# A shorter lag between scores and transposes in an attention loop, with the P·V matmuls regrouped, on one Trainium2 core

## The chip, the cores and the metric

The kernel runs on one core of one Trainium2 chip. The time is the device time of one execution in microseconds (us). Engines are named as in the profile: PE is TensorE's matmul, PEld its weight load, DVE is VectorE, ACT is ScalarE, POOL is GpSimd, SP issues most of the DMAs.

## The reference, cut to what matters

```python
scores = scale * q @ k.T + bias[h]          # 4 batches x 8 heads, 576 x 576, head size 64
attn = exp(scores - max); attn /= attn.sum(-1) + 1e-9
x = attn @ v                                # rows of 8 heads x 64 = 512
logits = x @ w_gate                         # 8 experts
noisy = logits + log1p(exp(x @ w_noise)) * noise
# the two best experts of each of 2304 rows, weights by softmax over the two
out[row] += weight * (relu(x[row] @ w1[e]) @ w2[e])
```

`bias` comes from a small network over the relative position; it is the same for all batches.

## The kernel before, in words

The program has three stages: the bias table (to about 65 us of the span), attention (about 65 to 345 us), and the routing and the expert layers (the rest). The change touches only attention.

There are 32 heads (4 batches of 8). The 576 query rows of a head are cut into five tiles, four of 128 rows and one of 64, so there are TILES = 160 tiles. One loop over t = 0..159 stands in the program of each engine (PE L606, DVE L809, ACT L1108), and each engine works its own list in order; semaphores tie the lists together.

In iteration t PE issues, in this order:

- `qk(t)` (L542): six matmuls give the scores of tile t in `ps[t % 2]`. It waits until DVE is through with tile t-2.
- `pv`: the output of one head is the sum over five key tiles kt of V times the transposed probabilities. `PVAT` maps (t - VLAG) mod 5 to the key tiles done in that iteration. Before, each iteration does one key tile (4 records at L599). VLAG = NU + LT + 1 is 12.
- `logits`: once in 40 iterations the gate matmuls of a whole batch (L581).
- `flip(t - LT)`, with LT = 6 (L560): transposes of the probabilities of tile t-6 into the PSUM banks `pt[0]` (first half of the rows) and `pt[1]` (second half). The fifth tile of a head uses one bank, the head's number mod 2.
- `xtile`: after the fifth tile of some heads, four transposes of finished outputs (L548), into the bank that the fifth tile leaves free.

`flip` has these two waits; `pt` has one buffer for each bank, so the second is for the copies of the flip before:

```python
pe.wait_ge(norm_done, t + 1)
for bank in banks(t):
    if uses(bank, ("p", t)):
        pe.wait_ge(t_done[bank], uses(bank, ("p", t)))
```

DVE does in iteration t `evac0(t - LT - 1)` (L796, the copy of `pt[0]` to SBUF, which increments `t_done[0]`), then `ttr(t)` (L775, bias, scale and row maximum), then, where (t-2) mod 5 is 1, 3 or 4, `recip(t - 2)` (L786 and L788). ACT does `evac1(t - LT - 1)` (L1084, the copy of `pt[1]`), `expo(t - 1)` (L1069) and once a head `oevac` (L1097, the head's output, at OLAG). POOL normalises each tile (`norm`, L1228) once `recip` is through, and between the norms it splits the q and k of the head after the next (`high` L1207 and L1209, `qlow` L1214, `klow` L1220). The probabilities lie in ER = 7 buffers `E`.

After the loop each engine has a hand-written order for the last flips, the last three heads' P·V, the gate matmuls and the start of the routing (PE L626 to L647, DVE L860 to L875, ACT L1128 onward).

Of the kernel before, what the change touches and what calls it, by code (L numbers as in the profile page):

```python
# [22 lines left out]
B, H, S, D = 4, 8, 576, 64  # L23
# [3 lines left out]
NU = -(-S // P)  # L27
# [57 lines left out]


TILES = B * H * NU
LT, ER = 6, 7
VLAG = NU + LT + 1
PVAT = {kt: (kt,) for kt in range(NU)}  # L90
OLAG = VLAG + max(PVAT) + 1
GLAG = OLAG + 1
XT = 96
# [6 lines left out]
def banks(t):  # L100

    n, u = divmod(t, NU)
    return (0, 1) if u < NU - 1 else (n % 2,)


def xtile_with(t):

    n, u = divmod(t, NU)
    if u < NU - 1 or n % H in (0, 4) or n < 5:
        return None  # L110
    b, at = divmod(n - 5, H)
    return b, at - (at >= NX)
# [16 lines left out]
def uses(bank, e):  # L129

    return ORDER[bank].index(e)


def xbank(b, u):

    return [("x", b, u) in o for o in ORDER].index(True)


def build(nc, qT, kT, v, rtab, pcol, rcp8, w1c, b1c, w2b, wg, noise, mw1, mw2, consts, out, xs):
    ctx = ExitStack()  # L140
    with ctx:
# [361 lines left out]
        def _(pe):  # L503
# [26 lines left out]
            def part(half):  # L530
                return slice(half * D, (half + 1) * D)
# [18 lines left out]
            def flip(t):  # L550

                n, u = divmod(t, NU)
# [4 lines that stand above are left out]
                for kt in range(NU):  # L557
                    for half in range(2 if u < NU - 1 else 1):
                        bank = half if u < NU - 1 else n % 2
                        mm = nc.tensor.transpose(pt[bank][:, kt * D:(kt + 1) * D], E[t % ER][part(half), kt * P:(kt + 1) * P],  # L560
                                                 ident[part(half), part(half)])
                        if kt == NU - 1:
                            mm.then_inc(t_ready[bank], 1)

            def flip_x(u, bank):

                group, c = divmod(u, NX)
                for j in range(4):
                    mm = tr(bank[0:XT, j * P:(j + 1) * P], OT[:, group * 4 + j, c * XT:(c + 1) * XT], P)
                return mm  # L570

            def xtile(b, u):
                bank = xbank(b, u)
                pe.wait_ge(ot_done, b * H + (u // NX + 1) * 4)
                pe.wait_ge(t_done[bank], uses(bank, ("x", b, u)))
                flip_x(u, pt[bank]).then_inc(t_ready[bank], 1)
# [8 lines left out]
            def pv(n, kts):  # L585
                b, h = divmod(n, H)
                if kts[0] == 0:
                    for t in (n * NU + NU - 2, n * NU + NU - 1):
                        for bank in banks(t):
                            pe.wait_ge(t_done[bank], uses(bank, ("p", t)) + 1)  # L590
                    pe.wait_ge(v_loaded[n % 4], 16 * (n // 4 + 1))
                    if n >= 2:
                        pe.wait_ge(ot_done, n - 1)
                    if h == 1 and b:
                        pe.wait_ge(g_done, b)

                for kt in kts:
                    for half in range(2):
                        mm = nc.tensor.matmul(po[half * D:(half + 1) * D, n % 2, 0:HALF], vs[n % 4][:, kt, :],  # L599
                                              PT[n % 2][:, kt, half * HALF:(half + 1) * HALF],  # L600
                                              start=kt == 0, stop=kt == NU - 1)
                        if kt == NU - 1:
                            mm.then_inc(pv_half, 1) if half == 0 else mm.then_inc(pv_done, 1)

            pe.wait_ge(pt_zeroed, 1)
            for t in range(TILES):  # L606
                qk(t)
                if t >= VLAG and (t - VLAG) % NU in PVAT:
                    pv((t - VLAG) // NU, PVAT[(t - VLAG) % NU])
                b, at = divmod(t - GLAG - (H - 1) * NU, H * NU)  # L610
# [12 lines left out]
                                          start=True, stop=True)  # L623
                mm.then_inc(lt_ready, 1)

            flip(TILES - 6)  # L626
            xtile(*xtile_with(TILES - 6))
            pv(B * H - 3, (3, 4))
            flip(TILES - 5)
            pe.wait_ge(ttr_done, TILES - 1)  # L630
            pe.wait_ge(g_done, B - 1)
            pe.wait_ge(pid_done, 2)
            folded(range(CL), 0)
            pv(B * H - 2, (0, 1, 2))
            flip(TILES - 4)
            pv(B * H - 2, (3, 4))
            flip(TILES - 3)
            pe.wait_ge(ttr_done, TILES)
            pe.wait_ge(ot_done, B * H - 2)
            logits(range(H - 2), ps[1][:, 0, :])  # L640
            flip(TILES - 2)
            pe.wait_ge(ot_done, B * H - 1)
            logits([H - 2], ps[1][:, 0, :])
            flip(TILES - 1)
            xtile(*xtile_with(TILES - 1))
            pv(B * H - 1, range(NU))
            pe.wait_ge(ot_done, B * H)  # L647
            logits([H - 1], ps[1][:, 0, :]).then_inc(g_ready, 1)
# [92 lines left out]
        def _(dve):  # L741
# [48 lines left out]
            def evac0(t):  # L790
                n, u = divmod(t, NU)
                dve.wait_ge(t_ready[0], uses(0, ("p", t)) + 1)
                if n >= 2:
                    dve.wait_ge(pv_half, n - 1)
                    dve.wait_ge(pv_done, n - 1)
                nc.vector.tensor_copy(PT[n % 2][:, :, u * P:u * P + D], pt[0][:, 0:NU * D].rearrange("p (k s) -> p k s", k=NU))\  # L796
                    .then_inc(t_done[0], 1)
# [61 lines left out]

            dve.wait_ge(p_loaded, 32)  # L860
            dve.wait_ge(c2_loaded, CONSTS2)
            evac0(TILES - 7)
            recip(TILES - 2)
            evac0(TILES - 6)
            recip(TILES - 1)
            evac0(TILES - 5)
            copied(early, 0)
            evac0(TILES - 4)
            perturbed(early, 0)
            evac0(TILES - 3)  # L870
            evac0(TILES - 2)
            indexed(early)
            x_evac(*xtile_with(TILES - 1))
# [146 lines left out]
        def _(act):  # L1020
# [56 lines left out]
            def evac1(t):  # L1077
                n, u = divmod(t, NU)
                at = u * P + (D if u < NU - 1 else 0)
                act.wait_ge(t_ready[1], uses(1, ("p", t)) + 1)  # L1080
                if n >= 2:
                    act.wait_ge(pv_half, n - 1)
                    act.wait_ge(pv_done, n - 1)
                nc.scalar.activation(PT[n % 2][:, :, at:at + D], pt[1][:, 0:NU * D].rearrange("p (k s) -> p k s", k=NU),  # L1084
                                     ACT.Copy).then_inc(t_done[1], 1)

            def oevac(n):
                b, h = divmod(n, H)
                act.wait_ge(pv_half, n + 1)
                act.wait_ge(pv_done, n + 1)  # L1090
                if h == 0 and b:
                    act.wait_ge(g_ready, b)
                if h % 4 == 0 and b:
                    for u in range(h // 4 * NX, h // 4 * NX + NX):
                        bank = xbank(b - 1, u)
                        act.wait_ge(t_ready[bank], uses(bank, ("x", b - 1, u)) + 1)
                nc.scalar.activation(OT[:, h, :], po[:, n % 2, 0:HALF], ACT.Copy).then_inc(ot_done, 1)  # L1097

            def x_evac(b, u):
                act.wait_ge(t_ready[1], uses(1, ("x", b, u)) + 1)  # L1100
                act.wait_ge(x_stored, 32 * b)
                nc.scalar.activation(*x_rows(u, pt[1]), ACT.Copy).then_inc(t_done[1], 1)

            def last_x(i, bank):
                act.wait_ge(x_ready, i + 1)
                nc.scalar.activation(*x_rows(NX + i, bank), ACT.Copy).then_inc(x_done, 1)
# [13 lines left out]
            def softplus(cs, half):  # L1120
                act.wait_ge(lt_copied, half + 1)
                some = ez[:, :, :].rearrange("p (a c) e -> p a c e", a=2)[:, :, cs[0]:cs[-1] + 1, :]
                raw = logit[:, :, NE:16].rearrange("p (a c) e -> p a c e", a=2)[:, :, cs[0]:cs[-1] + 1, :]
                nc.scalar.activation(some, raw, ACT.Exp).then_inc(r_act, 1)
                act.wait_ge(r_act, 2 * half + 1)
                nc.scalar.activation(some, some, ACT.Ln, bias=1.0).then_inc(r_act, 1)

            evac1(TILES - 7)  # L1128
            expo(TILES - 1)
            x_evac(*xtile_with(TILES - 6))  # L1130
            oevac(B * H - 3)
            evac1(TILES - 5)
            evac1(TILES - 4)
            softplus(range(CL), 0)
            oevac(B * H - 2)
            evac1(TILES - 3)
            evac1(TILES - 2)
            evac1(TILES - 1)
            oevac(B * H - 1)
            last_x(0, po[:, 1, :])  # L1140
            softplus(range(CL, NT // 2), 1)
# [232 lines left out]
```

## Time and profile before

| what | us |
|---|---|
| median of 3 runs | 859.82 (858.33 to 860.89) |
| the profiled execution | 859.82 |
| its span, first to last instruction | 858.0 |
| PE busy | 794.0 (93%) |
| DVE, ACT, POOL busy | 502.0, 391.9, 384.0 |
| from 100 to 327 us: PE busy | 227.0 of 227.0, granted clock 1.00 |
| from 100 to 327 us: DVE, ACT, POOL busy | 192.4, 169.8, 184.4 |

The span is cut into 40 slices of 21.45 us in the page; slices 4 to 15 are attention. An engine's share over the whole span mixes the three stages, so the stage has to be read by itself. The profiled execution lies 1.8 us over its span; that part is outside the first and the last instruction.

### The profile page before, as it was taken

What the parts mean: (1) busy time and instruction counts of PE and PEld (TensorE: products, weight loads), DVE (VectorE), ACT (ScalarE), POOL (GpSimd) and SP (SyncE); (2) the same over time, 40 slices, a digit from 0 to 9 for tenths busy, and PEclk for the clock granted to TensorE, in tenths of its full rate; (3) what the DMA queues carried; (4) which work ended last, traced back from release to release, by engine and by line L of the source; (5) the groups of instructions that cost most, each with busy time, mean ns of one, the idle gap of its engine ahead of it and who ended that gap; (6) DMA issues with size and microseconds to landing.
All of it is one profiled execution on the core that took longest, in us unless ns stands there. A gap on an engine that the chain in (4) does not pass through costs nothing.

```text
span 858.0 us, 18369 instructions
## 1 busy us (share of the span) xinstructions
PE 794.0 (93%) x6558; PEld 614.7 (72%) x6558; DVE 502.0 (59%) x1201; ACT 391.9 (46%) x824; POOL 384.0 (45%) x439
## 2 busy tenths in 40 slices
PE   3986999999999999249999999999999999999994
PEld 1335665666666665249899899898898998988983
DVE  5987888888888885883533524435336235344310
ACT  3996777777777774413423323234224123232200
POOL 4006888788787872053232432342333324412212
PEclk9998999999999999669999999999999999999998
DMA  6786343353343235244262470461643714712122
GB/s 137 205 229 147 100 117 89 93 154 87 98 142 100 83 114 210 59 131 189 50 169 103 75 245 12 77 231 33 129 157 56 213 49 73 246 14 37 14 25 37
DMA packets 51174, 97.16 MB, mean 113 GB/s; under 512 B 12640, under 2 KB 21472, under 8 KB 51104
## 3 DMA queue, kind: packets, MB, share of 16 engines
q1 hardware_dynamic: 39920, 74.55, 28.5%
q0 software_dynamic: 10320, 21.41, 13.6%
q8 instruction: 42, 0.69, 0.3%
q10 hardware_dynamic: 864, 0.29, 0.2%
q14 instruction: 28, 0.23, 0.1%
HBM read 65.07 MB, written 20.53 MB: 100 GB/s over the span
## 4 chain that ended last, share of the span: by engine, by line
PE 85%; DVE 4%; DMA 4%; ACT 2%; issue 2%; POOL 1%; SPq 1%; POOLq 0%; DVEq 0%; ACTq 0%
PE ps L704 26%; PE po L719 24%; PE po L599 12%; PE ps L542 8%; PE pt L560 8%; PE pt L548 3%; DMA out_rows<-ys,iscat 2%; PE ps L522 1%; ACT work L1052 1%; ACT work L1045 1%; DVE work L760 1%; PE po L522 1%; DVE ohlo L940 1%; DMA w2blk<-in_w2b 1%; DMA qraw<-in_qT 1%
## 5 line engine op out<-in xcount | busy, mean ns | idle before, releaser
L704 PE MATMUL ps<-xT,whi 128*128 128x320 f32 x1024 | 176.1, 309 | 1.0 <-ACT xT L1152 1.0
L719 PE MATMUL po<-whi,hT 128*128 128x512 f32 x640 | 162.5, 398 | 0.0
L1163 ACT ACTIVATE hT<-ps 128x320 fp32r<-128x320 f32 x128 | 56.0, 437 | 231.8 <-PE ps L704 231.8
L704 PEld LDWEIGHTS ps<-xT,whi 128*128 128x128 f32 x1024 | 156.2, 187 | 1.8 <-issue 1.2
L987 DVE SCALAR_TENSOR_TENSOR hT<-ps,hT 128x320 fp32r<-128x320 f32 x128 | 62.9, 492 | 153.0 <-ACT hT L1163 153.0
L1228 POOL TENSOR_SCALAR work<-work,rcp 128x576 f32<-128x576 f32 (+1 forms) x160 | 118.2, 748 | 51.2 <-DVE rcp L788 51.2
L719 PEld LDWEIGHTS po<-whi,hT 128*128 128x128 f32 x640 | 118.1, 188 | 26.9
L1267 POOL DMA_INDIRECT out_rows<-ys,iscat x40 | 68.5, 1712 | 133.3 <-DMA out_rows<-ys,iscat 75.3
L775 DVE CUSTOM_DVE_ANT_0 ns<-ps,slab 128x576 f32<-128x576 f32 (+1 forms) x160 | 120.8, 756 | 11.3 <-PE ps L542 11.1
L1069 ACT ACTIVATE work<-ns,nmax 128x576 f32<-128x576 f32 (+1 forms) x160 | 122.6, 766 | 3.8 <-DVE nmax L775 3.3
L560 PEld LDWEIGHTS pt<-cst,work 64*128 64x128 f32 x1440 | 62.7, 139 | 73.9 <-issue 42.8
L599 PE MATMUL po<-work,vs 128*64 128x288 f32 x640 | 112.0, 433 | 0.1
L1254 POOL DMA_INDIRECT xg<-x_rows,igath x30 | 32.4, 1081 | 153.3 <-DVE ys L1002 80.1
L1002 DVE TENSOR_SCALAR ys<-po,wrow 128x512 f32<-128x512 f32 x40 | 30.0, 751 | 112.9 <-PE po L719 102.3
L704 PE MATMUL ps<-xT,wlo 128*128 128x320 f32 x512 | 95.7, 308 | 0.0
L1084 ACT ACTIVATE work<-pt 128x320 f32<-128x320 f32 x144 | 63.0, 437 | 65.5 <-PE pt L560 64.1
L560 PE MATMUL pt<-cst,work 64*128 64x64 f32 x1440 | 84.2, 233 | 5.0 <-DVE work L796 2.1
L796 DVE COPY work<-pt 128x320 f32<-128x320 f32 x144 | 70.7, 491 | 26.9 <-PE pt L560 24.9
L719 PE MATMUL po<-wlo,hT 128*128 128x512 f32 x320 | 81.1, 395 | 0.0
L806 DVE TENSOR_TENSOR wlo<-wraw,whi 128x1024 fp32r<-128x1024 f32 x64 | 75.4, 1222 | 8.6 <-ACT whi L1074 8.6
L704 PEld LDWEIGHTS ps<-xT,wlo 128*128 128x128 f32 x512 | 80.3, 187 | 0.0
L719 PEld LDWEIGHTS po<-wlo,hT 128*128 128x128 f32 x320 | 60.0, 187 | 14.7
(132 smaller groups left out, 986.2 us busy)
## 6 DMA issues: line engine op xcount, KB each, us to landing
wraw<-in_mw SPq DMA_DIRECT2D x64, 512.0 KB, 9.5
slab<-work SPq DMA_DIRECT2D x36, 288.0 KB, 3.7
qraw<-in_qT SPq DMA_DIRECT2D x64, 144.0 KB, 2.8
vs<-in_v SPq DMA_DIRECT2D x32, 160.0 KB, 2.6
out_rows<-zeros SPq DMA_DIRECT2D x32, 152.0 KB
kraw<-in_kT SPq DMA_DIRECT2D x64, 72.0 KB, 2.5
x_rows<-xnat SPq DMA_DIRECT2D x8, 576.0 KB, 5.3
wrow<-w_rows,iscat POOLq DMA_INDIRECT x40, 2.4
```

Of the source, the lines that this page charges most:

```text
L542: mm = nc.tensor.matmul(ps[t % 2][:, half, 0:HALF], qq[n % 2][part(half), u * P:(u + 1) * P], kk[n % 2][part(half), :], start=i == 0, stop ...
L560: mm = nc.tensor.transpose(pt[bank][:, kt * D:(kt + 1) * D], E[t % ER][part(half), kt * P:(kt + 1) * P], ident[part(half), part(half)])
L599: mm = nc.tensor.matmul(po[half * D:(half + 1) * D, n % 2, 0:HALF], vs[n % 4][:, kt, :], PT[n % 2][:, kt, half * HALF:(half + 1) * HALF], ...
L704: mm = nc.tensor.matmul(bank, w1s[i][pw][:, c, f * P:(f + 1) * P], xT[px][:, c, half * HB:(half + 1) * HB], start=j == 0 and c == 0, stop= ...
L719: mm = nc.tensor.matmul(po[:, (i + t) % 2, :], hT[px][:, c, t * P:(t + 1) * P], w2s[i][pw][:, c, :], start=j == 0 and c == 0, stop=j == 2 ...
L775: nc.vector.tensor_tensor_reduce(out=ns[t % 2][0:r, :].rearrange("p (a s) -> p a s", a=2), in0=ps[t % 2][0:r, :, 0:HALF], in1=bias[0:r, u, ...
L796: nc.vector.tensor_copy(PT[n % 2][:, :, u * P:u * P + D], pt[0][:, 0:NU * D].rearrange("p (k s) -> p k s", k=NU))\
L806: nc.vector.tensor_tensor(wlo[i][:, c * WC:(c + 1) * WC], wraw[i][:, c * WC:(c + 1) * WC], whi[i][:, c * WC:(c + 1) * WC].bitcast(F32), AL ...
L1069: nc.scalar.activation(E[t % ER][0:r, 0:S], ns[t % 2][0:r, :], ACT.Exp, bias=nmax[0:r, i:i + 1], scale=-1.0, accum_out=ssum[0:r, i:i + 1]) ...
L1084: nc.scalar.activation(PT[n % 2][:, :, at:at + D], pt[1][:, 0:NU * D].rearrange("p (k s) -> p k s", k=NU), ACT.Copy).then_inc(t_done[1], 1)
L1228: nc.gpsimd.tensor_scalar(E[t % ER][0:r, 0:S], E[t % ER][0:r, 0:S], rcp[0:r, i:i + 1], 1.0, ALU.mult, ALU.mult)\
L1267: nc.gpsimd.indirect_dma_start(out=out, out_offset=bass.IndirectOffsetOnAxis(ap=iscat[:, t:t + 1], axis=0), in_=ys[i][:, :], in_offset=Non ...
```

## The change

The lag between the scores and the transposes goes from LT = 6 to 5 iterations, and the number of probability buffers from 7 to 6. With it VLAG goes from 12 to 11, OLAG from 17 to 16 and GLAG from 18 to 17. The P·V matmuls are no longer one key tile in each iteration: they are two, none, two, none and one key tile, in iterations with t mod 5 = 1, 2, 3, 4 and 0. The orders after the loop are rewritten to match.

```diff
-LT, ER = 6, 7
+LT, ER = 5, 6
-PVAT = {kt: (kt,) for kt in range(NU)}
+PVAT = {0: (0, 1), 2: (2, 3), 4: (4,)}
@@ PE, after the loop
-            flip(TILES - 6)
-            xtile(*xtile_with(TILES - 6))
-            pv(B * H - 3, (3, 4))
+            pv(B * H - 3, (4,))
             flip(TILES - 5)
+            pv(B * H - 2, (0, 1))
+            flip(TILES - 4)
...
             folded(range(CL), 0)
-            pv(B * H - 2, (0, 1, 2))
-            flip(TILES - 4)
-            pv(B * H - 2, (3, 4))
+            pv(B * H - 2, (2, 3))
             flip(TILES - 3)
+            pv(B * H - 2, (4,))
+            flip(TILES - 2)
...
             logits(range(H - 2), ps[1][:, 0, :])
-            flip(TILES - 2)
+            flip(TILES - 1)
+            xtile(*xtile_with(TILES - 1))
             pe.wait_ge(ot_done, B * H - 1)
             logits([H - 2], ps[1][:, 0, :])
-            flip(TILES - 1)
-            xtile(*xtile_with(TILES - 1))
             pv(B * H - 1, range(NU))
@@ DVE, after the loop
-            evac0(TILES - 7)
+            evac0(TILES - 6)
             recip(TILES - 2)
-            evac0(TILES - 6)
+            evac0(TILES - 5)
             recip(TILES - 1)
-            evac0(TILES - 5)
+            evac0(TILES - 4)
             copied(early, 0)
-            evac0(TILES - 4)
+            evac0(TILES - 3)
             perturbed(early, 0)
-            evac0(TILES - 3)
             evac0(TILES - 2)
@@ ACT, after the loop
-            evac1(TILES - 7)
+            x_evac(*xtile_with(TILES - 6))
             expo(TILES - 1)
-            x_evac(*xtile_with(TILES - 6))
+            evac1(TILES - 5)
             oevac(B * H - 3)
-            evac1(TILES - 5)
             evac1(TILES - 4)
+            evac1(TILES - 3)
             softplus(range(CL), 0)
-            oevac(B * H - 2)
-            evac1(TILES - 3)
             evac1(TILES - 2)
             evac1(TILES - 1)
+            oevac(B * H - 2)
             oevac(B * H - 1)
```

## Rows read from the trace of the kernel before

**Rows 1.** Busy time and granted clock by stretch; columns PE, PEld, DVE, ACT, POOL, clock.

```profile
206.75:214.43 7.68, 7.68 (x97) 4.70 (x96) 6.93 (x22) 5.92 (x16) 6.11 (x9) 1.00 0.36 102
214.43:217.07 2.64, 2.64 (x38) 1.35 (x36) 1.84 (x7) 1.74 (x6) 2.31 (x4) 1.00 0.35 104
```

**Rows 2.** Timeline of PE in the loop; start, duration, line, what, count.

```profile
208.29 0.53 PE L560 MATMUL pt<-cst,work 64*128 64x64 f32 x10
208.62 0.38 PE L542 MATMUL ps<-kh,qh 64*128 64x288 f32 x2
...
209.19 0.71 PE L599 MATMUL po<-work,vs 128*64 128x288 f32 x4
209.83 0.53 PE L560 MATMUL pt<-cst,work 64*128 64x64 f32 x10
...
211.37 0.40 PE L560 MATMUL pt<-cst,work 64*128 64x64 f32 x3
```

**Rows 3.** Timeline of DVE, then of ACT, behind the flip of 209.83.

```profile
210.39 0.49 DVE L796 COPY work<-pt 128x320 f32<-128x320 f32 x1 [0.30 <-PE pt L560]
...
210.42 0.44 ACT L1084 ACTIVATE work<-pt 128x320 f32<-128x320 f32 x1 [0.35 <-PE pt L560]
```

**Rows 4.** Timeline of PE as the loop fills, before the first P·V.

```profile
70.49 0.40 PE L542 MATMUL ps<-kh,qh 64*128 64x288 f32 x2 [0.43 <-DVE nmax L775]
...
70.99 0.47 PE L560 MATMUL pt<-cst,work 64*128 64x64 f32 x10
...
72.98 0.52 PE L560 MATMUL pt<-cst,work 64*128 64x64 f32 x10 [1.07 <-DVE work L796]
73.28 0.40 PE L542 MATMUL ps<-kh,qh 64*128 64x288 f32 x2
...
74.12 0.52 PE L560 MATMUL pt<-cst,work 64*128 64x64 f32 x10 [0.17 <-DVE work L796]
```

**Rows 5.** Timeline of DVE between the flips of 72.98 and 74.12.

```profile
73.51 0.49 DVE L796 COPY work<-pt 128x320 f32<-128x320 f32 x1
```

**Rows 6.** Timeline of PE after the loop's last scores.

```profile
325.62 0.38 PE L542 MATMUL ps<-kh,qh 64*128 64x288 f32 x2
...
326.82 0.53 PE L560 MATMUL pt<-cst,work 64*128 64x64 f32 x10
328.17 0.49 PE L560 MATMUL pt<-cst,work 64*128 64x64 f32 x5 [0.82 <-DVE work L796]
...
329.17 1.19 PE L599 MATMUL po<-work,vs 128*64 128x288 f32 x8
330.29 0.52 PE L560 MATMUL pt<-cst,work 64*128 64x64 f32 x10
330.75 1.52 PE L622 MATMUL ps<-fold,lacc 128*128 128x32 f32 x12
...
339.80 2.65 PE L599 MATMUL po<-work,vs 128*64 128x288 f32 x20
```

**Rows 7.** Timeline of POOL: the norms of a head's first two tiles.

```profile
208.94 1.47 POOL L1228 TENSOR_SCALAR work<-work,rcp 128x576 f32<-128x576 f32 x2 [1.00 <-DVE rcp L788]
```

**Rows 8.** Timeline of DVE and POOL: reciprocals' first step beside POOL's splits.

```profile
74.68 1.32 DVE L786 TENSOR_SCALAR sden<-ssum 128x2 f32<-128x2 f32 x1
...
74.55 1.42 POOL L1214 TENSOR_TENSOR ql<-qraw,qh 128x576 fp32r<-128x576 f32 x1
```

**Rows 9.** Timeline of PE at the first P·V.

```profile
81.79 1.23 PE L599 MATMUL po<-work,vs 128*64 128x288 f32 x4
82.95 0.79 PE L560 MATMUL pt<-cst,work 64*128 64x64 f32 x10
```

**Rows 10.** Busy time and granted clock by stretch, as in rows 1.

```profile
78.00:80.00 2.00, 1.34 (x15) 1.00 (x11) 1.73 (x5) 1.30 (x4) 2.00 (x5) 0.57 0.63 159
```

**Rows 11.** Timeline of DVE after the loop.

```profile
335.35 0.26 DVE L847 TENSOR_TENSOR work<-work,wnoise 128x96 f32<-128x96 f32 x1 [0.44 <-ACT work L1126]
...
336.89 0.49 DVE L796 COPY work<-pt 128x320 f32<-128x320 f32 x1
```

## The prediction

> **What bounds the kernel now.** I read the busy times by stretch first. From 100 to 327 us PE is busy for all 227.0 us at the full granted clock, 2.4 GHz (the table above). One head, five iterations, is 7.68 us: PE 7.68, DVE 6.93, ACT 5.92, POOL 6.11 [rows 1]. So in the loop the time is PE's list, and any other engine has 10% or more to spare.
>
> Then I read PE's own timeline for what one iteration is made of [rows 2]. From the start of one flip to the start of the next is 209.83 - 208.29 = 1.54 us: flip to scores 0.33, scores to P·V 0.57, P·V to flip 0.64. The reader should see that P·V stands between the scores and the flip in each iteration, and so gives the copies time. The flip's banks are copied at 210.39 by DVE and at 210.42 by ACT, 0.56 and 0.59 us after the flip's start [rows 3]; those copies end 1.05 and 1.03 us after it, and the next flip comes at 1.54. At present the wait for them costs nothing, with 0.49 us in hand.
>
> **The change part by part.**
>
> *Two key tiles in one iteration.* After the loop there is a P·V of two key tiles: 329.17 to the flip at 330.29 is 1.12 us, against 0.64 for one [rows 2, 6]. The second costs 0.48, so going in and out of P·V costs 0.16 each time. Two of five entries go; with the 0.07 that the scores reach a flip sooner than a P·V (0.50 below, 0.57 above) that is -0.46 a head, if nothing else happens.
>
> *Iterations without P·V.* There the list is flip, scores, flip. Its instructions need 0.33 to the scores and 0.50 from the scores to the flip (70.49 to 70.99) [rows 2, 4], so 0.83. But the flip writes the one buffer of each bank, and waits for both copies of the flip before. The fill of the loop shows exactly this pattern: flip at 72.98, scores at 73.28, DVE's copy from 73.51 to 74.00, and the flip at 74.12, its wait put down to that copy [rows 4, 5]. That is 1.14 us from flip to flip. In the loop I put it together as 0.56 to the copy, 0.49 for it, and 0.11 from its end to the flip (74.00 to 74.12 is 0.12): 1.155. ACT's copy gives 0.59 + 0.44 + 0.11 = 1.14, no later. Is DVE free at that time? It is busy for 6.93 of 7.68 us a head [rows 1], and the new pattern puts the three `recip` into the three iterations that have P·V, so that it has idled for some tenths before both light flips. So 1.155 it is, with 1.14 as the near bound, 0.83 as the lower one if the copies did not bind, and 1.35 as the upper one: 326.82 to 328.17 is another flip that waits for a copy [rows 6].
>
> *The cycle.* A flip that has waited starts on an idle PE, and the scores follow it after 0.30 (72.98 to 73.28), not 0.33 [rows 4]. The double iteration is then 0.305 + 0.57 + 1.12 = 1.995. A head: 2×1.995 + 2×1.155 + 1.54 = 7.84, against 7.68. It comes out 0.16 slower: some 0.62 us of waiting for copies against 0.46 saved. From t = 14 to 158 there are 29 such cycles: +4.6 us. Each 0.01 on the light iteration is 0.58 us of the total.
>
> *Gate matmuls.* An iteration with them takes 2.64 us [rows 1], 1.10 more than one without. They fall into a light iteration now, where the copies end meanwhile: 0.33 + 0.57 + 1.10 = 2.00, in place of the 1.155 + 1.10 = 2.255 that the cycle above and 1.10 would give. Three batches, -0.7 us.
>
> *LT from 6 to 5, and six buffers.* The norm of a tile must be done one iteration sooner. Two norms run from 208.94 to 210.41 [rows 7], so the first tile is ready at 209.68. Its flip was the one after that of 211.37 [rows 2] and becomes that of 211.37, 1.7 us after the norm. By the same count the other tiles of a head have 1.6 us or more. The six buffers wait for the same flip relative to LT. No cost. `high`, `qlow` and `klow` keep their place on POOL, SP's loads hang on them as before, and `oevac`, the bank of `po` and V's loads all move by one iteration together with P·V.
>
> *The fill.* The scores of t = 10 are held by POOL's split for the third head, which hangs on a DMA; the change doesn't touch it. From 78 us the granted clock is near half (0.57 from 78 to 80 us [rows 10]: the 1.2 GHz level for most of it), after a stretch of waits. Before, P·V begins at t = 12: 81.79 to 82.95 is 1.16 us for one key tile at this clock [rows 9], 1.8 times the 0.64. After, it begins at t = 11 with two, 1.16 + 0.48×1.8 = 2.03, of which 0.7 fills a wait for DVE that PE had there: +1.3 us. t = 12 sheds its P·V and waits for a copy: +0.1 by then. t = 13 has two, at a clock that comes back in it: +0.6 to +0.9. I take +0.7 us, for one flip and one key tile more done by then.
>
> *After the loop.* From the last scores (325.62) to the last head's P·V (339.80) is 14.18 us [rows 6]. After, from the last scores: flip 154 at 0.83, its x tile, one key tile from 1.83; flip 155 would come at 2.47 but bank 1 is copied late (x tile at 1.28, its end and the copy 1.38 later), 2.66; two key tiles from 3.11, flip 156 at 4.23; the folded matmuls from 4.69, 1.45 (their 1.52 [rows 6] less an overlap of 0.07); two key tiles, flip 157 at 7.26; one key tile, flip 158 at 8.43, held 0.08 by a copy; gate matmuls from 8.88, flip 159 at 9.97. Its x tile waits for `evac0(158)`, which DVE has behind the first part of the routing: that takes 336.89 - 335.35 = 1.54 us [rows 11] from about 8.92, then the copy, so 11.06. Then 0.57 for the x tile, 0.60 for the gate of one head, P·V at 12.25. That is -1.9 us. What follows is the same code in the same state; its copies of expert weights run with slack.
>
> **Sum.** 859.8 (the profiled execution, which is also the median) + 4.6 - 0.7 + 0.7 - 1.9 = 862.5 us.
>
> **What the skill says on it.** The fill shows a 1.32 us `sden` of DVE [rows 8] that stands still until POOL's 1.42 us split beside it ends. The Trainium skill, SBUF — State Buffer, "SBUF: two separate sides", has it that these two engines share a port pair which the first taker holds for its whole instruction; the trace agrees. By that rule a moved `recip` could be held in each head. I place the `sden` of a head's first two tiles 4.3 us after the reciprocal before it, and the end of `klow` 4.4 us after that (two norms, a split of 1.42, a norm, a split), so the hold is 0.1 us, with 0.4 us of DVE slack behind it; the sum stays.
>
> **The rivals.**
>
> *A, the copies don't bind.* If a light iteration took 0.83 us, 58 of them would give 58 × 0.325 = 18.9 back: 843.6 us. For it: PE would be busy throughout, as now. Against it: the wait in the code and the flip of 74.12 in rows 4.
>
> *B, not slower: the fill keeps its clock.* The clock falls at 78 us, after PE has waited for much of the fill [rows 4, 10]. With an earlier first flip PE has more to do just there. If the clock stayed up, the iterations of t = 11 and 12 would take 1.54 us each instead of 1.8 times that for most of them, 2.1 us less, and the 0.7 above goes: 859.7 us. It decides as soon as no stretch after 78 us shows the lower clock; against it, the DMA and the splits that PE waits for stay.
>
> *C, more is late at the light flips.* If a light iteration took the 1.35 us of rows 6, because DVE or ACT comes to the copy late, that is 58 × 0.195 = 11.3 more: 873.8 us. For it: DVE has only 0.75 us a head to spare. Against it: the `recip` are elsewhere.
>
> *D, the clock falls inside the loop.* PE now idles 0.3 us twice a head. An iteration at 1.2 GHz takes 1.8 × 1.54 = 2.8 us [rows 9]; an episode of two or three, as in the fill, costs some 3 us, and one in each batch 12: 874.5 us. Against it: the fall of rows 10 follows waits of 1.07 us and more [rows 4]. The Trainium skill, TensorE: Matmul & The Clock Gate, "A second HAM failure mode: psum-queue depth-cycling", describes short PE idles between groups that make the clock go back and forth; no row in the loop before shows it.
>
> **How the numbers follow.** Likeliest 62% (862.5, own range 860 to 866, from 1.14 to 1.20 for the light iteration and 1 us each on fill and tail), A 10%, B 16%, C 8%, D 4%. A measurement of this kernel can tell about 0.3%, 2.6 us, from no change. The likeliest lies on that line: 32 points slower, 29 same, 1 faster. A is faster; B is 13 same and 3 faster; C and D are slower. That is 0.14 faster, 0.42 same, 0.44 slower. The range leaves out A, and most of C and D: 858.5 to 868.
>
> **What would show it.** In the profile after: flips 1.15 us apart in light iterations with waits for L796 or L1084, some 0.3 us each, and PE's busy share in the loop down from 100% to about 92%; doubles of 2.0 us; five iterations in 7.84 us; the last scores 4.6 us later and the last head's P·V 12.3 us after them. Five iterations under 7.6 us would prove the central step wrong, and over 8.0 would mean C or D.

## The result and the profile after

The changed kernel is slower: 865.4 us median of ten executions against 860.5, a ratio of 1.0067 (95% interval 1.0047 to 1.0088). The forecast was 862.5, slower by 2.7 us; the profiled execution took 862.81 us (span 861.0), 3.0 us over that of before. Where the other 1.9 us of the medians come from is taken up further down. One execution of a later variant (e7) took 1109.17 us at a mean clock of 0.655 and is left out of that variant's median.

A light iteration is one without P·V, a double one has two key tiles, a single one has one. The rows are one head in the loop, the iteration with the gate matmuls behind it, and the first light iteration of that head; columns as in [rows 1]:

```profile
207.49:215.41 7.92, 7.50 (x97) 4.91 (x95) 6.76 (x22) 5.88 (x16) 6.82 (x10) 1.00 0.34 97
215.41:217.42 2.01, 2.01 (x34) 1.16 (x33) 1.28 (x4) 1.26 (x4) 2.01 (x3) 1.00 0.04 12
207.49:208.66 1.17, 0.98 (x18) 0.77 (x17) 0.64 (x3) 0.64 (x3) 1.17 (x2) 1.00 0.03 7
```

Five iterations are 7.92 us, where [rows 1] had 7.68, and PE is no longer busy throughout (95% from 100 to 320 us, 209.9 of 220.0). The iteration with the gate matmuls is 2.01 us and has no wait. PE's timeline in the first light iteration, then DVE's and ACT's beside it, answer to [rows 2] and [rows 3]:

```profile
207.49 0.52 PE L560 MATMUL pt<-cst,work 64*128 64x64 f32 x10
...
208.66 0.53 PE L560 MATMUL pt<-cst,work 64*128 64x64 f32 x10 [0.20 <-DVE work L795]
208.97 0.41 PE L542 MATMUL ps<-kh,qh 64*128 64x288 f32 x2
...
209.57 1.19 PE L599 MATMUL po<-work,vs 128*64 128x288 f32 x8
210.69 0.52 PE L560 MATMUL pt<-cst,work 64*128 64x64 f32 x10
...
211.89 0.37 PE L560 MATMUL pt<-cst,work 64*128 64x64 f32 x3 [0.22 <-DVE work L795]
```

```profile
208.05 0.49 DVE L795 COPY work<-pt 128x320 f32<-128x320 f32 x1 [0.53 <-PE pt L560]
```

```profile
208.08 0.44 ACT L1082 ACTIVATE work<-pt 128x320 f32<-128x320 f32 x1 [0.53 <-PE pt L560]
```

The scores end early and PE stands until the copy (208.05 to 208.54) is through; the flip comes at 208.66, 1.17 us after the one before. Both engines had idled for 0.53 us before they could copy, so in this trace it is the chain flip, copy, flip that is too long, and no engine's load; the experiment with shorter copies below tests it. The waits of the stretch from 100 to 320 us, grouped (who for whom, total, times, longest), hold two lines that the kernel before did not have:

```profile
PE pt L560 <- DVE work L795: 7.4, 36, 0.2
PE pt L560 <- ACT work L1082: 2.6, 13, 0.2
```

After the loop, PE from the last scores to the last head's P·V, for [rows 6]:

```profile
330.66 0.38 PE L542 MATMUL ps<-kh,qh 64*128 64x288 f32 x2
...
331.53 0.49 PE L560 MATMUL pt<-cst,work 64*128 64x64 f32 x5 [0.22 <-DVE work L795]
...
341.69 0.61 PE L548 MATMUL pt<-cst,OT 128*96 128x128 f32 x4 [0.44 <-DVE work L795]
...
342.84 2.65 PE L599 MATMUL po<-work,vs 128*64 128x288 f32 x20
```

From the last scores to the last head's P·V that is 12.18 us against 14.18.

### The profile page after: what moved, and what is told of

It reads as the page before. It is cut to its first block, busy times and chain, and to the rows that moved or that the text cites. A ratio compares the mean times of both kernels' runs of the same rounds, so it can differ in the third digit from the quotient of the medians.

```text
span 861.0 us, 18370 instructions
## 1 busy us (share of the span) xinstructions
PE 789.1 (92%) x6558; PEld 620.7 (72%) x6558; DVE 496.6 (58%) x1201; ACT 389.4 (45%) x824; POOL 383.1 (44%) x439
## 3 DMA queue, kind: packets, MB, share of 16 engines
q0 software_dynamic: 10320, 21.41, 13.6%
## 4 chain that ended last, share of the span: by engine, by line
PE 80%; DVE 7%; DMA 4%; ACT 4%; issue 3%; SPq 1%; POOL 0%; POOLq 0%; DVEq 0%; ACTq 0%
PE ps L703 26%; PE po L718 23%; PE po L599 11%; PE pt L560 9%; PE ps L542 5%; PE pt L548 3%; DVE work L795 3%; DMA out_rows<-ys,iscat 2%; ACT work L1043 2%; ACT work L1050 1%; DVE work L759 1%; DMA slab<-work 1%; ACT work L1082 1%; DVE ohlo L938 1%; DMA qraw<-in_qT 1%
## 5 line engine op out<-in xcount | busy, mean ns | idle before, releaser
L1264 POOL DMA_INDIRECT out_rows<-ys,iscat x40 | 68.1, 1702 | 134.1 <-DMA out_rows<-ys,iscat 79.7
L599 PE MATMUL po<-work,vs 128*64 128x288 f32 x640 | 99.2, 424 | 0.0
```

Source lines behind the costliest of these rows:

```text
L1264: nc.gpsimd.indirect_dma_start(out=out, out_offset=bass.IndirectOffsetOnAxis(ap=iscat[:, t:t + 1], axis=0), in_=ys[i][:, :], in_offset=Non ...
```

## The experiments

**The two halves of the change.** The first keeps everything but the grouping, the second keeps only the grouping.

```diff
-PVAT = {0: (0, 1), 2: (2, 3), 4: (4,)}      # e1: the changed kernel with
+PVAT = {kt: (kt,) for kt in range(NU)}
```

> The shorter lag, six buffers and the new order after the loop, but P·V with one key tile in each iteration as before. Theory (the loss is the light iterations, which wait for the copies of pt): a head takes 7.68 to 7.69 us again, no flip in the loop waits for L795 or L1082, the last head's P·V comes 12.2 us after the last scores (14.2 before), and the time is 857.5 to 859.5 us. The changed kernel's executions lie in two groups, near 862.5 us at a mean clock of 0.973 and near 867.5 us at 0.965 to 0.970. If the idle PE of the light iterations is what loses the clock, this kernel has the first group only; if the fill or the order after the loop does it, it shows the second group too, some 5 us higher. Rival (the shorter lag itself costs, by norms that come late): a head over 7.75 us with waits for POOL at the flips.

Measured: 858.79 us, 0.9971 (0.9951 to 0.9992) of before. Flips stand 1.54 us apart as before, the stretch from 100 to 200 us has PE busy for all of it, and the last head's P·V comes 12.5 us after the last scores (325.40 to 337.94; I expected 12.2, and 0.44 of it is the x tile's wait). The lag costs nothing in the loop; what it gains lies after it. Four of the twelve executions lie at 860.4 to 862.4 us and the others at 857.1 to 859.0, some 3 us apart and not the 5 of the theory.

```diff
-PVAT = {kt: (kt,) for kt in range(NU)}      # e2: the kernel before with
+PVAT = {0: (0, 1), 2: (2, 3), 4: (4,)}
-            pv(B * H - 3, (3, 4))
+            pv(B * H - 3, (4,))
```

> Lag 6, seven buffers and the order after the loop of before, but the key tiles grouped two, none, two, none, one (one key tile fewer is left for after the loop). Theory: light iterations of 1.17 to 1.20 us and doubles of 2.02, a head of 7.92 to 7.95 us, so some +6 us in the loop and nothing gained after it (13.7 us from the last scores to the last head's P·V): 864 to 868 us at a clock of 0.973, and with some executions about 5 us higher if the light iterations lose the clock. Rival (grouping saves its switches and the loss is elsewhere): a head under 7.6 us and 848 to 856 us.

Measured: 868.18 us, 1.0065 (1.0041 to 1.0088). Its flips from 207.57 stand 2.03, 1.17, 2.03, 1.19 and 1.51 us apart, 7.93 a head. The grouping alone makes the loss, with either lag, and the rival of saved switches is out. Two details missed: the median of the seven executions (867.3 to 869.4) lies just over the 864 to 868 us expected, and the last head's P·V comes 14.58 us after the last scores (330.70 to 345.28) and not 13.7. In its profile the clock came back only after the experts had begun (386.4), and from there to the end it took 479.6 us, against 477.4 before.

**The copies made shorter.** Both copies of `pt` take two of the five key tiles, and P·V reads those in place of all five; the rest of the probabilities is left out. Only the times in the loop can be compared, so the time of its one execution, 852.96 us, says nothing on the change.

```diff
-nc.vector.tensor_copy(PT[n % 2][:, :, u * P:u * P + D], pt[0][:, 0:NU * D]...
+nc.vector.tensor_copy(PT[n % 2][:, 0:KC, u * P:u * P + D], pt[0][:, 0:KC * D]...   # KC = 2; L1082 likewise
```

> The changed kernel with the two copies of pt cut to two of the five key tiles (the rest of the probabilities is left out, and P·V reads those two only); the routing then sees other values, so that only the attention loop's times are to be read. Theory: a copy takes 0.25 to 0.3 us instead of 0.49, and each light iteration gets as much shorter, 1.17 to 0.93 to 1.0 us, a head 7.92 to 7.45 to 7.6 us. Rival (the light iteration is held by something other than the copies, as the normalisation or the switch between kinds of matmul): light iterations stay at 1.17 us and a head at 7.9.

Flips in its loop, light (154.10 to 155.12), double, light (157.15 to 158.14):

```profile
154.10 0.52 PE L561 MATMUL pt<-cst,work 64*128 64x64 f32 x10
155.12 0.52 PE L561 MATMUL pt<-cst,work 64*128 64x64 f32 x10
157.15 0.52 PE L561 MATMUL pt<-cst,work 64*128 64x64 f32 x10
158.14 0.49 PE L561 MATMUL pt<-cst,work 64*128 64x64 f32 x5
```

```profile
206.75 0.29 DVE L796 COPY work<-pt 128x128 f32<-128x128 f32 x1 [0.42 <-PE pt L561]
```

The copy takes 0.29 us, 0.20 less, and the light iterations take 1.02 and 0.99, 0.15 to 0.18 less, while the doubles stay at 2.03. A head without an x tile takes 7.56 us (from the flip of 168.67 to that of 176.23), in the expected 7.45 to 7.6. A light iteration follows the copy's length: that it is the copies is shown, not only read off a releaser. Had it all of the 0.20 it would be 0.97 to 1.00; what keeps the rest of up to 0.05 us is open.

**Where the executions differ.** The executions of either kernel lie in two groups 4 to 5 us apart. In the changed kernel's they go with the mean clock: 861.5 to 864.6 us at 0.972 to 0.976, and 866.0 to 869.6 us at 0.964 to 0.970. Single key tiles in the first three heads were to show whether the fill makes them:

```diff
+                kts = SINGLE if n < 3 else PVAT
```

> The changed kernel with one key tile in each iteration for the first three heads and the grouping from the fourth on. Theory (the extra 5 us of some executions come from the light iterations in the loop): the executions lie in the same two groups, near 862 and 867 us. Rival (they come from the fill, where the clock falls and comes back): one group only, near 862 us, mean clock 0.973 or more.

Measured: 866.52 us, 1.0041 (1.0024 to 1.0058); 11 of 12 at 865.8 to 867.2. Neither expectation fits: the groups did not stay as they were, and what is left is the upper one. That speaks for the fill having a part in it and does not say how. Its profile has a stretch at half clock of 17 us in the fill (67.6 to 84.7), where the changed kernel's has 6.8 (74.4 to 81.3).

> The changed kernel, unaltered, beside the kernel before and the variants on one chip. The loop is to repeat: a head 7.92 us, the last head's P·V 12.2 us after the last scores. Theory on the 2 us that the medians show beyond the 3.0 us of the two first profiles: they come from the length of the two stretches at 1.2 GHz (the fill, and the handover from the routing to the experts), which vary from execution to execution in both kernels; so its executions lie between 862 and 869 us with the mean clock falling from 0.973 to 0.964 as the time rises, and its median stays 3 to 7 us over that of before. Rival (the light iterations lose the clock): the profile shows a stretch at 0.5 between 100 and 320 us.

Measured: 865.19 us, 1.0044 (1.0019 to 1.0069), seven executions at 862.8 to 865.3 (0.970 to 0.974) and five at 867.5 to 870.6 (0.963 to 0.967). The loop and what follows it repeat: a head of 7.93 us (205.79 to 213.72) and the last head's P·V 12.18 us after the last scores (330.99 to 343.17). Beside it the kernel before had 35 executions: 17 at 859.1 to 861.6 and 18 at 862.5 to 866.2. In no profile of any kernel here is there a stretch at half clock between 100 and 320 us, so the light iterations don't lose the clock there; that rival is out. Two of these profiles, of e2 and e4, are of executions of the upper group's time (867.85 and 867.18 us); of the two kernels themselves no execution of the upper group was profiled. Lower group against lower group the medians of the two kernels are 2.3 us apart in the first result and 4.3 here. How often an execution falls into the upper one varied with the chip: one at most of the ten of before (862.82) and five of the ten of the changed kernel in the first result, 18 of 35 and 5 of 12 here. Whether the change itself alters the share is open.

**One wait less after the loop, and a busy handover.** The handover is the stretch between the last head's P·V and the first matmul of the experts. PE builds two lists there that say which row goes to which expert (the second is L674, 36 matmuls, 11.3 us of waiting after the first), then transposes the gathered rows. The variants e7 to e9 give PE matmuls of constants to do in that wait; nothing reads their results.

```diff
             copied(early, 0)                  # e6, on e1
             evac0(TILES - 3)
+            evac0(TILES - 2)
             perturbed(early, 0)
-            evac0(TILES - 2)
```

> The shorter lag with single key tiles, and after the loop DVE's copy of flip 158 ahead of the first part of the routing. Theory: the x tile after flip 159 no longer waits for that copy (0.44 us in the changed kernel), the last head's P·V comes 11.6 to 11.8 us after the last scores, and the time is 0.4 to 0.6 us under that of the variant with the shorter lag alone, 857.5 to 859 us. Rival (the routing's part, 0.5 us later, becomes what is late): the last P·V earlier, but the gate's later steps and the experts' first matmul no earlier against it.

Measured: 858.08 us, 0.9956 (0.9936 to 0.9977). The last P·V comes 12.4 us after the last scores (325.65 to 338.04), not 11.7: the x tile no longer waits, but the gate of one head behind it now waits for the head's output on ACT (`337.44 ... [0.25 <-ACT OT L1095]`), so nearly all of it was handed on.

```diff
             mm.then_inc(lista_ready, 1)       # e7, on e6
+            for _ in range(6):
+                nc.tensor.matmul(ps[1][:, 1, :], ones, cst[:, 0:512], start=True, stop=True)
```

> As the variant with the copy first, plus six fp32 matmuls of constants (128x512, results unused) on PE between the first and the second list of rows, where PE waits for some 11 us. Theory (executions differ by where the clock comes back at the handover): the clock is at 1.00 before the second list's matmuls, these take 1.3 to 1.6 us instead of 2.5 and the first transposes 0.63 instead of 1.10, so that the experts begin 1.5 to 2.5 us earlier, and the executions lie closer together: median 854 to 857 us. Rival (the filler matmuls run into the wait for the second list, or hardly move the clock): no faster than 857.5 us, or slower.

Measured: 860.88 us (eleven executions, 857.1 to 863.6), 0.998 (0.9958 to 1.0002), so the rival. The clock came back at 364.7, was lost at 371.5 and returned at 385.1, with the second list begun at 373.1 and the experts at 380.3; the second list took 2.46 us, as without them.

> The changed kernel with the same six matmuls. Theory (handover): its median falls by 3 to 5 us against the unaltered one beside it, more than the 1.5 to 2.5 us that the matmuls save in an execution with an early clock, and its upper group goes. Rival (the fill makes the groups): the two groups stay 4 to 5 us apart, each 1.5 to 2.5 us lower.

Measured: 866.45 us, 1.0048 (1.0027 to 1.0069), not under the 865.19 of the unaltered one, so neither the theory nor the rival came true. Six filler matmuls end 4.6 us before the next work in e7's profile and 3.2 us before it here, and no gain is measured in either kernel.

> The copy-first variant with eleven filler matmuls instead of six. With six, the filler ended at 368.5 us, the clock had come back at 364.7 and was lost again at 371.5, before the second list of rows at 373.1. Theory (the clock at the handover costs what the executions differ by): eleven reach to about 373 us, the clock stays at 1.00 into the experts, the second list takes 1.3 to 1.6 us instead of 2.46, the first transposes 0.63 instead of 1.1, the experts begin 1.5 to 2.5 us earlier against the first scores, and the time is 854 to 857 us. Rival (the filler is in the way, or the clock falls all the same): the second list starts later than the copy-first variant's, counted from the last head's P·V, and the time is 858 us or more.

PE's timeline at this handover, then that of the copy-first variant without filler:

```profile
361.42 11.09 PE L672 MATMUL ps<-cst 128*128 128x512 f32 x22
372.89 1.49 PE L676 MATMUL pt<-rhsb,ohlo 128*128 128x75 f16 x36 [0.39 <-DVE rhsb L956]
...
378.81 1.41 PE L705 MATMUL ps<-xT,whi 128*128 128x320 f32 x4 [0.90 <-ACT xT L1151]
```

```profile
372.10 2.46 PE L674 MATMUL pt<-rhsb,ohlo 128*128 128x75 f16 x36 [11.34 <-DVE rhsb L954]
...
378.77 0.82 PE L703 MATMUL ps<-xT,whi 128*128 128x320 f32 x4 [0.87 <-ACT xT L1149]
```

Measured: 858.6 us, 0.9957 (0.9938 to 0.9977), so by the time the rival. The second list does take 1.49 us instead of 2.46 and the first transposes 0.62 instead of 1.10 (374.22 and 374.36), but the experts begin only 0.8 us sooner, 39.97 us after the last P·V against 40.73, and in this profile the clock went down again at 377.9, after the waits for the gathered rows, so that their first matmuls run at half speed (1.41 us for what takes 0.82) until 384.7. In this profile the gain at one place is given back at the next; over the executions it lies 1.0 us under the copy-first variant on the same chip (e10, below), which the intervals do not tell from nothing.

> The copy-first variant again, on the same chip as the shorter lag alone: 0.4 to 0.6 us under it in the lower group of executions, 0.995 to 0.998 of the kernel before.

Measured: 859.63 us, 0.9971 (0.9948 to 0.9994).

> The shorter lag with single key tiles again: 0.996 to 0.999 of the kernel before, some 6.5 us under the changed kernel's 865.2.

Measured: 859.57 us, 0.9969 (0.9948 to 0.999). The copy-first order is no better than the lag alone; both are faster than the kernel before, by 0.3%, and with it than the changed one. The 0.3% is small, but the intervals leave out 1; the shorter way after the loop gives 1.6 to 1.8 us in the profiles (12.4 to 12.6 us against 14.18).

The profile of e10 happened on an execution that never left the full clock in the fill, and got it back late at the handover (at 382.4, with the experts begun at 377.0):

```profile
66.00:90.00 24.00, 19.22 (x250) 12.79 (x250) 20.91 (x66) 18.24 (x46) 19.12 (x26) 1.00 0.53 128
```

```profile
66.00:90.00 24.00, 21.86 (x226) 15.53 (x223) 18.90 (x60) 16.67 (x43) 17.92 (x25) 0.72 0.50 115
```

(The second is the repeated changed kernel, at a mean of 0.72.) With it the last head's P·V came at 335.86 us where the same program had it at 338.04: the half clock of the fill is worth some 2 us. Six profiles are of programs that are alike up to the last scores, and from the first scores to the last they took 258.4 us with no half clock in the fill (e10), 260.6 with 10.2 us of it (e11), 260.9 and 261.2 with 13.6 (e6, e1), 261.4 and 261.6 with 17.1 (e7, e9).

From the experts' first matmul to the end e10 took 479.9 us, with the clock back 5.4 us after that matmul; with the clock back before it, it took 477.4 (before, after, e1) and 477.5 (e6). That is another 2.4. The others agree: 478.4 to 478.8 us with the clock back 3 to 4 us after that matmul (e4, e5, e11), 479.6 to 480.2 with about 5 to 6 us (e2, e7, e8, e9).

The two places together have the size of the distance between the groups. That they make the groups is argued from these profiles, one for each run, and not shown: I did not control which group an execution falls into. Part of the spread is no matter of the clock either: in most executions some 1.8 to 2.0 us lie outside the span, in some 3.0 or more (e4's and e10's profiled ones, 7 of 29 of before on the last chip).

## Why the prediction was right, step by step

The sign and the mechanism held: the light iterations wait for the copies, and the shorter end takes back part of the loss. Two terms of the sum were off, the other way round, and what parts the executions was not in it.

- *Light iteration, 1.155 forecast:* 1.17, and 1.20 into the fifth tile of a head. The 0.11 us from the end of a copy to the flip measured 0.12 (208.54 to 208.66), and 0.15 before the fifth tile (211.74 to 211.89).
- *Double, 1.995 forecast:* 2.03 and 2.02. I had let the flip that waited give 0.03 us back before the scores, for both doubles. Only one of the two follows such a flip. There it does (208.66 to 208.97 is 0.31), but the way from those scores to P·V is 0.60, not 0.57, so it is gone again.
- *Single, 1.54 forecast:* 1.50, as it too follows a flip that waited.
- *The cycle:* a head is 7.92, not 7.84: 0.06 more on the two light iterations, 0.06 on the two doubles, 0.04 less on the single. That is a head without an x tile. In 19 of the 29 an x tile follows the fifth tile; with it a head went from 8.41 to between 8.62 and 8.65. Over the 29 cycles the loop term was +6.6, where I had +4.6. This is the step that was mis-sized.
- *The signs at the flips:* the waits are 0.20 to 0.22 us, not 0.3, and PE's share is 95%, not 92%. The 0.83 us that I set against 1.155 runs to the point where a next flip could start; the scores themselves end 0.98 us after the flip (208.18 and 0.29), and only what follows counts as idle. The time lost is the same.
- *Gate matmuls, -0.7:* 2.01 us for 2.00; set against the real light iteration it is -0.8.
- *From the scores of t = 14 to the last,* all terms together: 325.62 - 85.75 = 239.87 before, 330.66 - 85.02 = 245.64 after, +5.8 against the +3.9 forecast.
- *The fill, +0.7:* -0.1. From the first scores to those of t = 14 it took 85.02 - 64.61 = 20.4 us, against 85.75 - 65.22 = 20.5. The work is as forecast, the double P·V at t = 11 took 1.96 us at half clock (79.53 to 81.49), but the clock had gone at 74.4 and was back at 81.3 where I had left it down until 85.4. This is half of rival B, and by chance of the execution: the same program had 13.6 us of half clock there in e5, not 6.8.
- *After the loop, -1.9:* -2.0, with flip 154 at 0.87, the x tile held by the copy behind the routing's first part for 0.44, P·V at 12.18 us.
- *The shorter lag costs nothing:* shown by e1, which has no wait at a flip in the loop.
- *DVE and POOL's shared port, a hold of 0.1 us:* `sden` of two tiles lasts 0.15 to 0.17 us everywhere in the loop after (from 80 us on), so even that was not paid there. In e3 it lasts 0.27 to 0.29 us in most heads (at 156.81 beside POOL's split of 156.27 to 157.06), and no flip in its loop is put down to a wait for DVE. The rule is that of the Trainium skill (SBUF — State Buffer, "SBUF: two separate sides"), that the first taker keeps the shared pair for its whole instruction; e3's trace agrees.
- *Rival D:* no profile shows the clock below full between 100 and 320 us, with PE waiting twice a head. The Trainium skill describes a clock that goes back and forth with short idles of PE (TensorE: Matmul & The Clock Gate, "A second HAM failure mode: psum-queue depth-cycling"); with waits of 0.20 to 0.22 us here it did not set in.
- *Before the first scores* the two profiled executions differ by -0.6 us, which no part of the change explains; in e5 the same program had its first scores another 0.6 us earlier (63.98).

The sum by the profiles: -0.6 - 0.1 + 5.8 - 2.0 = 3.1, against 3.0 measured and 2.7 forecast. That the total came so close is luck: the loop and gate terms were 1.9 us too low, and the fill and the time before the first scores gave 1.4 back. What the forecast did not have at all is that the time of this kernel falls into two groups; three executions of before (858.3 to 860.9) didn't show it. Half of the changed kernel's ten executions and one at most of the kernel before's lie in the upper group, and that is likely most of the difference between +3.0 in the profiles and +4.9 in the medians; it is not shown.

## What to carry to other kernels

On the engine that sets the time, merging two visits to a matmul kind saved the switch here (a double P·V to its flip is 1.12 us, two singles are 2 × 0.64), but it also takes away work that hid somebody's latency. Before moving such work, add up the shortest chain through each single buffer (here flip, copy, flip: 1.17 us) and compare it with what remains between the two uses (0.83 by the prediction's rows). Judge a change with two halves by running each alone: here one was worth -0.3% (0.9971 alone) and the other cost some 0.7 to 1.0% (1.0065 alone, and 1.0044 to 1.0067 against 0.9971).

## What the runs showed of the hardware that I had not expected

- The granted clock fell at different times in the fill of the same program (66.0 for 10.2 us and 79.7 for 3.4 us in one execution of the changed kernel, 74.4 for 6.8 us in another). Of the copy-first program, one execution was at half clock for 13.6 us of the fill (e6) and another not at all (e10).
- Eleven filler matmuls brought the clock back in a stretch where PE otherwise waits 11.3 us, and it was lost again after two waits of 0.7 to 1.1 us and the shorter work between them; the same sequence without filler had kept, through waits of 0.61 and 0.87 us, a clock that returned at 376.2 (e6).
- A copy from PSUM to SBUF of 128x320 took DVE 0.49 us and one of 128x128 0.29: by a straight line through these two, an estimate, 0.10 us for each 96 columns on some 0.16 that don't depend on the size.
